# Attention with routed experts: the gate's products move behind those with v, the turnings of x behind those of the next q and k

## What is computed

```python
scores = scale * q @ k.T - log(S)          # q, k, v: (4, 12, 448, 64)
x = sigmoid(scores) @ v                    # then (1792, 768): tokens x (heads, 64)
logits = x @ w_gate                        # (1792, 8)
# pairs (token, expert) in falling order of logit; a token takes the first expert
# that still has room (cap = 1792 // 8 = 224 tokens each)
out[mask_e] = relu(x[mask_e] @ w1[e]) @ w2[e]
h = out @ w_in                             # w_in: 768 x 2048
y = (max(h, 0) + alpha * min(h, 0)) @ w_out
```

## Time and profile before

| | |
|---|---|
| median of 3 runs | 1049.4 us (1048.82 to 1050.76) |
| the profiled execution's own time | 1050.24 us |
| its span, first to last instruction | 1048.6 us |
| TensorE's matmuls busy | 996.9 us, 95% of the span |
| VectorE, ScalarE, GpSimd busy | 54%, 37%, 18% |
| mean granted clock of TensorE | 0.989 |
| attention stage | start to about 200 us |

### The profile page before, as it was taken

How to read it: one execution, slowest core, us unless ns; L and a number is a source line. 1 busy time by engine, 2 the same in 40 slices (tenths; PEclk the granted TensorE clock), 3 DMA queues, 4 the chain that set the end, 5 groups by cost and what they waited for, 6 DMA issues and landing times.

```text
span 1048.6 us, 16652 instructions
## 1 busy us (share of the span) xinstructions
PE 996.9 (95%) x6515; PEld 854.9 (82%) x6515; DVE 568.6 (54%) x1289; ACT 392.6 (37%) x629; POOL 189.4 (18%) x202
## 2 busy tenths in 40 slices
PE   7999999988969999999999999999999999999994
PEld 5555555558968898799989999998999999999993
DVE  4344444698646828947862774695458546211110
ACT  5677667301331123346222225641121455222213
POOL 0011001114520011234201025440101336000001
PEclk9999999999989999999999999999999999999998
DMA  9999995416588576766878846578785446966501
GB/s 209 273 267 276 264 282 189 166 40 228 176 249 292 193 225 191 262 173 197 308 267 225 258 160 153 178 253 337 231 237 189 145 133 189 395 222 212 180 1 53
DMA packets 121475, 222.32 MB, mean 212 GB/s; under 512 B 51424, under 2 KB 69216, under 8 KB 121408
## 3 DMA queue, kind: packets, MB, share of 16 engines
q1 hardware_dynamic: 87152, 120.11, 36.7%
q0 software_dynamic: 21280, 91.59, 28.0%
q10 hardware_dynamic: 12976, 9.70, 3.9%
HBM read 184.84 MB, written 36.52 MB: 211 GB/s over the span
## 4 chain that ended last, share of the span: by engine, by line
PE 84%; DVE 9%; issue 2%; ACT 2%; DMA 1%; POOL 0%; DVEq 0%; POOLq 0%; ACTq 0%
PE psum L947 19%; PE psum L935 19%; PE psum L912 11%; PE psum L882 11%; PE psum L674 8%; PE psum L658 6%; DVE hits L1460 4%; PE psum L877 2%; PE psum L642 2%; PE psum L685 1%; PE psum L907 1%; DMA stage<-x_rows,tok_idx 1%; PE psum L829 1%; DVE unit L1360 1%; PE psum L693 1%
## 5 line engine op out<-in xcount | busy, mean ns | idle before, releaser
L947 PE MATMUL psum<-g_high,unit 128*128 128x448 f32 x768 | 231.1, 369 | 4.5 <-DVE g_low L1388 4.3
L935 PE MATMUL psum<-y_high,unit 128*128 128x448 f32 x768 | 230.8, 368 | 4.4 <-ACT below L1089 4.3
L947 PEld LDWEIGHTS psum<-g_high,unit 128*128 128x128 f32 x768 | 144.3, 188 | 19.1 <-DVE g_low L1388 7.9
L935 PEld LDWEIGHTS psum<-y_high,unit 128*128 128x128 f32 x768 | 144.3, 188 | 17.8 <-ACT below L1089 5.8
L947 PE MATMUL psum<-g_low,unit 128*128 128x448 f32 x384 | 140.3, 365 | 0.0
L935 PE MATMUL psum<-y_low,unit 128*128 128x448 f32 x384 | 140.3, 365 | 0.0
L1360 DVE TENSOR_TENSOR unit<-raw,unit 128x768 fp32r<-128x768 f32 (+1 forms) x106 | 110.1, 1061 | 53.3 <-ACT unit L1062 45.2
L912 PE MATMUL psum<-h_high,unit 128*128 128x224 f32 x672 | 118.1, 279 | 10.9 <-issue 10.9
L1088 ACT ACTIVATE above<-psum 128x448 f32<-128x448 f32 x64 | 35.0, 547 | 248.2 <-PE psum L935 248.2
L1383 DVE SCALAR_TENSOR_TENSOR below<-below,neg_alpha,above 128x448 f32<-128x448 f32 x64 | 43.8, 684 | 146.7 <-ACT below L1089 146.6
L882 PE MATMUL psum<-x_high,unit 128*128 128x224 f32 x672 | 117.3, 276 | 0.0
(11 more groups left out here) (173 smaller groups left out, 1303.3 us busy)
## 6 DMA issues: line engine op xcount, KB each, us to landing
unit<-ffn_parts SPq DMA_DIRECT2D x120, 768.0 KB, 6.4
ffn_parts<-pre_parts POOLq DMA_DIRECT2D x24, 768.0 KB, 6.8
ffn_parts<-unit SPq DMA_DIRECT2D x8, 768.0 KB, 6.1
q_in<-in_q_dram SPq DMA_DIRECT2D x24, 224.0 KB, 5.3
v_in<-in_v_dram SPq DMA_DIRECT2D x24, 224.0 KB, 7.2
x_rows<-x_tok POOLq DMA_DIRECT2D x8, 672.0 KB, 6.0
rank_in<-suit_flat POOLq DMA_DIRECT2D x6, 896.0 KB
k_in<-in_k_dram SPq DMA_DIRECT2D x23, 224.0 KB, 7.1
```

Source lines behind the costliest of these rows:

```text
L935: last = pe.matmul(psum[:, IN_BANK, 0:PAIR], w, y[:, c, :], start=(c == 0 and i == 0), stop=(c == DC - 1 and i == 2))
L947: last = pe.matmul(psum[:, OUT_BANK + d, 0:PAIR], w, g[:, m % 2, :], start=(m == 0 and i == 0), stop=(m == FC - 1 and i == 2))
```

## The change

TensorE: in each step the gate's products move from behind the turnings of q and k to behind the products with v at the step's end, and the turnings of x take the place that they leave. The gate's products now go to the first 112 columns of TB, the bank of the turned rows of x (of the last pair still to O). So `turn_x` waits for the gate sum of the pair before (`gate_added`), a wait that `attend` loses; and `gate` waits for `copy_x` of its own pair. VectorE: `copy_x` moves from behind `copy_xT` to behind `split_qk`, ahead of `split_pre`, and `add_gate` from the step's start to behind `copy_xT`.

```diff
@@ bank
-        O_GATE = O[:, 0:P]
+        O_GATE, TB_GATE = O[:, 0:P], TB[:, 0:P]
@@ TensorE, attend
                     pe.wait_ge(xT_copied, xT_out(n - 1))
-                    pe.wait_ge(gate_added, gate_of(n - 1))
@@ TensorE, turn_x
                 pe.wait_ge(xT_copied, xT_out(n))
                 pe.wait_ge(x_copied, x_out(n - 1))
+                pe.wait_ge(gate_added, gate_of(n - 1))
@@ TensorE, gate
-            def gate(b, hp):
+            def gate(b, hp, to):
                 pe.wait_ge(xT_copied, xT_out(pair(b, hp)))
+                if to is TB_GATE:
+                    pe.wait_ge(x_copied, x_out(pair(b, hp)))
                 for j in range(JT):
-                    last = pe.matmul(O_GATE[GATE_ROWS * j:GATE_ROWS * j + E], w_gate_sb[:, hp, :],
+                    last = pe.matmul(to[GATE_ROWS * j:GATE_ROWS * j + E], w_gate_sb[:, hp, :],
@@ TensorE, work_on
                     turn_qk(*at(i + 2))
                 if not first:
-                    gate(*at(i - 1))
+                    turn_x(*at(i - 1))
...
                 attend(*at(i), range(JT - 1, JT))
                 if not first:
-                    turn_x(*at(i - 1))
+                    gate(*at(i - 1), TB_GATE)
@@ TensorE, behind the last batch
-            gate(B - 1, PAIRS - 1)
+            gate(B - 1, PAIRS - 1, O_GATE)
@@ VectorE, work_on
-                if not first:
-                    add_gate(*at(i - 1), last_batch)
                 if not last_batch or i + 2 < PAIRS:
                     split_qk(*at(i + 2), 0)
                     split_qk(*at(i + 2), 1)
                 if not first:
+                    copy_x(*at(i - 1))
                     split_pre(*at(i - 1))
                 if last_batch and i == PAIRS - 1:
                     early_values()
                     split_pre(b, i)
                 copy_xT(*at(i))
                 if not first:
-                    copy_x(*at(i - 1))
+                    add_gate(*at(i - 1), last_batch, TB_GATE)
```

More of the change, by code:

```diff
@@ L1208, in copy_x, with add_gate @@
                                 TB[0:P, :].rearrange("p (j d) -> p j d", j=JT)).then_inc(x_copied, 1)
-            def add_gate(b, hp, constant):
+            def add_gate(b, hp, constant, sums):
                 n = pair(b, hp)
                 here = gate_sums[:, b:b + 1, :] if constant else gate_sums[:, bass.ds(b, 1), :]
-                part = O_GATE.unsqueeze(1)
+                part = sums.unsqueeze(1)
                 dve.wait_ge(gate_done, gate_of(n))
@@ L1345, in _ @@
                 work_on(B - 1, i, False, True)
-            add_gate(B - 1, PAIRS - 1, True)
+            add_gate(B - 1, PAIRS - 1, True, O_GATE)
             def split_sel(r, piece):
```

## The result

The changed kernel takes 1050.64 us (median of 20 runs, 1049.46 to 1054.16), the kernel before 1048.8 us in the same comparison (20 runs, 1047.32 to 1050.96). The ratio is 1.0017, with a 95% interval of 1.0010 to 1.0025: **1.8 us slower, between 1.0 and 2.6**. That is inside the 0.2% (2.1 us) named ahead as the same, though the interval reaches a little over it; the forecast was +1.7.

What follows compares the result with a forecast made beforehand. TensorE's own order was taken to bound the attention stage. The terms 0 + 0.1 + 0.28 + 0.46 + 0.87 = +1.7 us, added to a median of 1049.4, gave 1051.1 us; range 1049.7 to 1053.2.

Steps and rivals of the forecast that it cites:

- The regular step at 0: Steps 2 to 19 and 20, 21: only TensorE's order changes, three changes of tile stay three, price 0 per step.
- The slack of 0.02: Regular step: the load of x's turnings can go at +1.02 after copy and gate sum, and is due at +1.04.
- Steps 20 and 21 at +0.1: Both follow a written-out copy starting 0.22 behind the first load, not 0.12, and lose about 0.05 us each.
- Step 1 at +0.28: First step: x's turnings replace the gate and wait for the copy; scores start at 23.61 instead of 23.33.
- Step 22 at +0.46: Last batch: x's turnings wait for the copy and the gate's sum; scores start at 186.73 instead of 186.27.
- Step 23 and the suits at +0.87: End of attention: VectorE's copy of x's rows, ahead of split and early suits, starts the split at 194.84, not 193.97.
- the 0.32: Last step of attention: products with v start at 194.44 instead of 194.12, a delay counted inside the 0.87.
- The sum and the end: Whole kernel: terms total +1.7 us, first turnings of the suits at 199.5, and the chain behind passes the delay on.
- the sum of the gate holds every step: Regular steps: x's turnings wait for `gate_added`, 20 x 0.1 = 2.0 us more, 1053.1 us, slower; chance 0.2.
- v to gate costs nothing: Regular steps: the gate starts 0.1 earlier, of which 0.04 a step is gained, 0.8 in all, 1050.3 us; chance 0.08.
- Another phase of the clock: Second experts' matmuls behind TensorE's stall: a shifted slow-clock stretch, 2.65 us, gives 1047.1 or 1053.1 us; chance 0.12.
- The change does nothing: End of attention: the last step's chain has unseen cover, so 0.87 goes, 1050.2 us; chance 0.08.

Runs made afterwards that it cites:

- the run with a fourth: Kernel before with the gate's products between the turnings of q and those of k, one more change of tile per step: 1053.42 us, ratio 1.0031.
- three idle copies: Changed kernel with three unused VectorE copies between the copy of the products with v and the gate's sum in every step: 1055.89 us, ratio 1.0053.
- The two delays: Kernel before with 16 or 32 dependent VectorE copies ahead of the first expert's search: 1055.15 us, ratio 1.0051, and 1058.0 us, ratio 1.0068.

## Why the prediction was right

The verdict (the same, by the bound of 0.2%), the size (+1.7, measured +1.8) and the place (the ends of the stage, not the loop) came out as forecast. That 1.7 lies so close to 1.8 is partly luck: the terms measured in the trace add up to 2.05, which the interval of 1.0 to 2.6 holds as well. The 1051.1 was 0.5 above the 1050.64 measured, since it started from a median of three runs (1049.4) that lay 0.6 above that of twenty (1048.8). Point by point:

- **The regular step at 0.** Right. All its starts came at the predicted positions, and the period grew by 0.008, which makes 0.14 in 17 steps that the sum had at nothing. The three changes of tile keep their number; the run with a fourth gives the price of one, 0.156, above the some 0.1 that the prediction ascribed to the array, a share for which it had no row.
- **The slack of 0.02.** Right in sign, too small: the sum starts 0.54 after its copy and not 0.57, so the load has 0.07, and some 0.03 more lies behind it, since the load can be that late before the scores are.
- **Steps 20 and 21 at +0.1.** Measured +0.13. The load of x's turnings starts 1.14 behind the gate's there (178.06 to 179.20), not 1.04, and 0.12 behind the end of the sum (178.82 + 0.26), so the sum holding it fits, although the list of waits has no entry for it.
- **Step 1 at +0.28.** Mis-sized: +0.45. The term at fault is the release from the copy to the load, for which I took 0.06 from step 22; it was 0.22. In step 1 the wait that ends last is that for the copy, and the loop has it on a register instruction ahead of the turnings (L684). In steps 22 and 23, which are written out, the release was 0.11 (186.67 + 0.26 = 186.93 to 187.04) and 0.12. In the loop with three idle copies, where the wait for the sum stands on the turnings themselves, it was 0.04. That the register instruction is the cause was not tested by itself, and one run speaks against it: with the old order in step 1, the loop's step 2 was held by the wait for `copy_x`, which the changed kernel has on the same register instruction, and its load went 0.07 behind that copy's end (30.69 to 30.76). So the 0.22 is measured and its cause is open.
- **Step 22 at +0.46.** Measured +0.45 for the step, with errors that nearly cancel: the release was 0.11 instead of 0.06, the turnings took 0.58 instead of 0.60, so the scores start 1.49 behind the copy (before 1.01), 0.48 later and not 0.46.
- **Step 23 and the suits at +0.87.** Measured +0.88. The run with `copy_x` behind the early suits took 0.77 of it away, so it was this copy and the wait for its turnings. That the 0.32 is inside the 0.87 held too.
- **The sum and the end.** The terms give 2.05 instead of 1.7. By the wording of the prediction's last part the suits were to start at 199.5; they start at 200.00, of which 0.15 were lost before the change begins and 0.17 in step 1. The two delays support that what is late here is late at the end.

The rivals: *the sum of the gate holds every step* did not happen, by 0.07 us; its mechanism is shown by the three idle copies. *v to gate costs nothing* fell: with it the gate would start 0.1 earlier than x's turnings did, and both start 0.90 behind v's first load. *Another phase of the clock*: the 144 matmuls behind the stall took 18.65, before 18.72, and 17.9 to 19.3 in the other profiles; no step of 2.65 was seen, and the rival has no support in these profiles. *The change does nothing* fell with the accounting of the steps.

## What to carry to other kernels

Where one engine's own order is the time of a loop, as here, reordering its work moved nothing (0.008 a step) and can be expected to move nothing unless it changes the number of changes of tile or lets a wait through; price each change of tile (0.156 here) and the slack of each new wait, and leave the loop. The cost of such a change lies at the irregular ends: the first step, the steps in which the work that gave cover is missing, and an operation put ahead of a serial chain, which costs its length and the wait for its own input (0.88 here, for a copy of 0.69). And an order tested in some steps only is another kernel, with seams of its own where two orders share a bank.

## What I had not expected

- A small VectorE copy listed with 0.21 us, queued between two others, moved the next operation by only 0.12; three of them moved the sum to start 0.92 behind its copy instead of 0.54, so 0.13 each.
- From the end of VectorE's work to TensorE's load behind it: 0.04 to 0.06 in the loop where the three idle copies held it, 0.07 at the seams, 0.11 in step 22, 0.22 in step 1.
- TensorE's stall between the second experts' products scatters from 7.1 to 9.6 us between single profiles, with the transfers at full rate (388 and 397 GB/s in the two windows shown). A span from one profile is no measure of a change of 2 us; the starts of each step are, to some 0.1 us.
